# First MoE of a three-stage kernel: where the down products, the low part of the weights' sums and the copies of y stand in each engine's order

## The reference, cut to what matters

```python
attn = attention(q, k, v, tau)                # 32 heads of 576 x 64, thresholded softmax
x = attn.transpose(0, 2, 1, 3).reshape(2304, 512)
a = x @ w_a                                   # first MoE: 512 -> 1536, twice
b = x @ w_b
y = a * b @ w_out                             # 1536 -> 512
h = y @ w_in                                  # second MoE: 512 -> 1024
solu = h * softmax(h)
out = (layernorm(solu) * g_ln) @ w_out2       # 1024 -> 512
```

## Time and profile before

| | |
|---|---|
| median of 3 executions | 1001.8 us (1001.01 to 1002.4) |
| the profiled execution | 1002.01 us |
| its span, first to last instruction | 999.8 us |
| PE busy | 953.1 us (95%) |
| DVE busy | 806.3 us (81%) |
| POOL busy | 631.4 us (63%) |
| ACT busy | 509.5 us (51%) |
| first MoE, chunks 1 to 4, on PE | from 381 to 780 us |

### The profile page before, as it was taken

How to read it: one execution, slowest core, us unless ns; L and a number is a source line. 1 busy time by engine, 2 the same in 40 slices (tenths; PEclk the granted TensorE clock), 3 DMA queues, 4 the chain that set the end, 5 groups by cost and what they waited for, 6 DMA issues and landing times.

```text
span 999.8 us, 18862 instructions
## 1 busy us (share of the span) xinstructions
PE 953.1 (95%) x6222; PEld 877.2 (88%) x6222; DVE 806.3 (81%) x1298; ACT 509.5 (51%) x823; POOL 631.4 (63%) x570
## 2 busy tenths in 40 slices
PE   5999999999999998998899989998999989999998
PEld 4999999999998997998899879997999777888886
DVE  6788788878778577888788877888899778888884
ACT  3777777777778554333433343334343643333332
POOL 2777777777778346777467756775888654443320
PEclk9999999999999999999899999999999999999999
DMA  6666666666763843221311131213210200000001
GB/s 176 160 161 164 157 157 157 159 161 159 168 150 101 235 159 89 67 82 65 84 63 63 63 92 59 79 63 129 82 65 22 85 1 32 32 21 21 21 21 43
DMA packets 55676, 96.66 MB, mean 97 GB/s; under 512 B 15576, under 2 KB 24408, under 8 KB 55632
## 3 DMA queue, kind: packets, MB, share of 16 engines
q1 hardware_dynamic: 55632, 96.10, 35.1%
HBM read 58.41 MB, written 5.32 MB: 64 GB/s over the span
## 4 chain that ended last, share of the span: by engine, by line
PE 82%; DVE 8%; ACT 3%; DMA 3%; issue 2%; POOL 1%; SPq 1%; DVEq 0%; POOLq 0%; ACTq 0%
PE PS L1654 12%; PE PS L1616 8%; PE PS L1681 8%; PE PS L1618 8%; PE PS L1683 8%; PE PS L1682 8%; PE PS L1776 4%; PE PS L1777 4%; PE PS L1778 4%; PE PS L1857 3%; PE PS L1859 3%; PE PS L1858 3%; PE PS L1800 2%; PE PS L1802 2%; PE PS L1801 2%
## 5 line engine op out<-in xcount | busy, mean ns | idle before, releaser
L660 POOL TENSOR_TENSOR p_lo<-prob,p_hi 128x576 fp32r<-128x576 f32 x144 | 208.7, 1451 | 49.9 <-ACT p_hi L853 48.0
L1681 PE MATMUL PS<-x_parts,w_parts 128*128 128x256 f32 x672 | 198.1, 295 | 20.3 <-DVE w_parts L1353 20.3
L1616 PE MATMUL PS<-ops 128*128 128x288 f32 x642 | 181.6, 304 | 14.4 <-DVE ops L1269 6.7
L1683 PE MATMUL PS<-x_parts,w_parts 128*128 128x256 f32 x672 | 193.5, 288 | 0.0
L1682 PE MATMUL PS<-x_parts,w_parts 128*128 128x256 f32 x672 | 193.4, 288 | 0.0
L1618 PE MATMUL PS<-ops 128*128 128x288 f32 x642 | 177.0, 297 | 0.0
L1189 DVE TENSOR_REDUCE neg_max<-PS 128x1 f32<-128x576 f32 x144 | 108.4, 755 | 59.7 <-PE PS L1618 59.6
L1681 PEld LDWEIGHTS PS<-x_parts,w_parts 128*128 128x128 f32 x672 | 132.4, 197 | 25.0 <-issue 18.2
L1616 PEld LDWEIGHTS PS<-ops 128*128 128x128 f32 x642 | 122.2, 190 | 23.3 <-issue 12.0
L728 POOL TENSOR_TENSOR w_parts<-w_raw,w_parts 128x768 fp32r<-128x768 f32 x48 | 90.5, 1885 | 80.1 <-ACT w_parts L980 80.1
L1682 PEld LDWEIGHTS PS<-x_parts,w_parts 128*128 128x128 f32 x672 | 132.6, 197 | 1.5
(11 more groups left out here) (170 smaller groups left out, 2287.7 us busy)
## 6 DMA issues: line engine op xcount, KB each, us to landing
w_raw<-w_ab_dram SPq DMA_DIRECT2D x60, 512.0 KB, 3.4
qk_raw<-qkT_dram SPq DMA_DIRECT2D x32, 288.0 KB, 3.0
ops<-qk_hi SPq DMA_DIRECT2D x62, 144.0 KB
ops<-qk_hi SPq DMA_DIRECT2D x31, 288.0 KB
ops<-qk_lo SPq DMA_DIRECT2D x62, 144.0 KB
v_raw<-v_tiles_dram SPq DMA_DIRECT2D x32, 160.0 KB, 2.7
xT<-head_sb SPq DMA_DIRECT2D x32, 144.0 KB, 3.1
out_dram<-o_sb SPq DMA_DIRECT2D x18, 256.0 KB, 2.0
```

The source lines that it names most:

```text
L660: pool.tensor_tensor(p_lo[:, s, :], prob[:, s, :], p_hi[:, r, :].bitcast(F32), ALU.subtract).then_inc(p_lo_done, 1)
L1616: pe.matmul(ps[:, b, 0:HALF], weights[0][:, r, own], moving[0][:, r, cols], start=(n == 0), stop=False)
L1681: pe.matmul(up_ps(bank, half), w[:, 0, :], x[:, 0, :], start=(k == 0), stop=False)
L1683: ins = pe.matmul(up_ps(bank, half), w[:, 1, :], x[:, 0, :], start=False, stop=(k == 1))
```

## The change

Nothing is computed otherwise; instructions change places.

- **PE**: `down(c, 11)` goes behind `up(c + 1, 0)` of the next chunk. `down(c, 8)` is cut into two halves (two banks each), one behind `up(c, 9)`, the other behind `up(c, 10)`. `down(c, 9)` and `down(c, 10)` stay behind `up(c, 11)`. Chunk 0 keeps its order but for its `down(0, 11)`.
- **DVE**: `low_sums` of the next tile stands behind the third of the nine operations of `products`, instead of behind the ninth. At f = 11, `low_x_block(., 0)` and `low_x_sums(., 0)` stand ahead of `low_gates`.
- **ACT**: at f = 11, `high_x_block(., 1)` stands ahead of `high_gates`, with part 0.
- **ACT and DVE**: `y_out(c - 1)` follows the gate of tile 0 of chunk c.
- **PE, ACT, DVE**: chunk 1 is written out, the loop runs over chunks 2 and 3.
- **Hand-over**: ACT does three blocks of `high_wout` ahead of `expo_step(0, 0)` instead of six, two ahead of the last `y_out`, two behind the copy that follows, one behind `high_normed(0, 0)`. POOL's `low_wout` is spread in a like way.

```diff
@@ POOL
-            low_wout(range(5))
+            low_wout(range(3))
             low_y(1, (0, 1))
+            low_wout(range(3, 4))
             pool.wait_ge(half_set, 1)
             rstd(0, 0)
             low_y(1, (2, 3))
-            low_wout(range(5, 7))
+            low_wout(range(4, 7))
@@ ACT, later_step
                 if f == NF - 1 and not final:
                     high_x_block(c + 1, 0)
+                    high_x_block(c + 1, 1)
                 high_gates(c, f)
+                if f == 0:
+
+                    y_out(c - 1)
                 if f == NF - 1 and not final:
-                    for part in range(1, 4):
-                        high_x_block(c + 1, part)
+                    high_x_block(c + 1, 2)
+                    high_x_block(c + 1, 3)
                     high_blocks(c + 1, 1)
@@ ACT, loops
-            y_out(0)
-            with act.Fori(1, NCH - 1) as c:
+            for f in range(NF):
+                later_step(1, f)
+            with act.Fori(2, NCH - 1) as c:
                 for f in range(NF):
                     later_step(c, f)
-                y_out(c)
@@ ACT, hand-over
-            high_wout(range(6))
+            high_wout(range(3))
             act.wait_ge(y_done, LAST + 9)
             expo_step(0, 0)
             high_y(1, (0,))
             act.wait_ge(y_done, LAST + 10)
             expo_step(0, 1)
             high_y(1, (1, 2))
-            high_wout(range(6, NK2))
+            high_wout(range(3, 5))
             y_out(NCH - 1, range(NK))
             copy_first(1)
+            high_wout(range(5, 7))
 
             act.wait_ge(wout_lo, 2)
             high_normed(0, 0)
+            high_wout(range(7, NK2))
@@ DVE, products
                 done(dve.tensor_tensor(up_3[:, :], up_ps(1, 1), up_2[:, :], ALU.add))
+
+                if f + 1 < NF:
+                    low_sums(c, f + 1)
+                elif not (isinstance(c, int) and c == LAST_CHUNK):
+                    low_sums(c + 1, 0)
                 dve.wait_ge(up_part, 3 * m + 3)
@@ DVE, later_step
                 products(c, f)
-                if f + 1 < NF:
-                    low_sums(c, f + 1)
-                    low_gates(c, f)
-                elif not final:
+                if f == NF - 1 and not final:
                     low_x_block(c + 1, 0)
-                    low_gates(c, f)
-                    low_sums(c + 1, 0)
                     low_x_sums(c + 1, 0)
+                low_gates(c, f)
+                if f == 0:
+                    y_out(c - 1)
+                if f == NF - 1 and not final:
                     low_x_sums(c + 1, 1)
                     low_x_block(c + 1, 1)
-                else:
-                    low_gates(c, f)
@@ PE
-            def down(c, f, split=False):
+            def down(c, f, split=False, ms=range(NK)):
...
+            def chunk(c, split=False, last=False):
+
+
+                for f in range(NF):
+                    up(c, f)
+                    if f == 0:
+                        down(c - 1, NF - 1, split)
+                    elif f < NF - 3:
+                        down(c, f - 1)
+                    elif f < NF - 1:
+                        half = (f - (NF - 3)) * NK // 2
+                        down(c, NF - 4, ms=range(half, half + NK // 2))
                 if not last:
-                    for f in range(NF - 3, NF):
-                        down(c, f, split)
+                    for f in range(NF - 3, NF - 1):
+                        down(c, f)
```

More of the change, by code:

```diff
@@ L1034, in _ @@
                     high_x_block(1, 0)
+                    high_x_block(1, 1)
+                    high_sums(1, 0)
                 high_gate(f)
@@ L1038, in _ @@
                     high_wo(f + 2)
-            high_x_block(1, 1)
-            high_sums(1, 0)
             high_x_block(1, 2)
@@ L1319, in first_gate, with low_sums @@
                 dve.tensor_tensor(gate[:, 0:H], gate[:, 0:H], PS[:, 2 * (f % 2) + 1, 0:H], ALU.mult).then_inc(g_done, 1)
+            def low_sums(c, f):
+                m = NF * (c - 1) + f
+                dve.wait_ge(w_hi_done, NF + 2 * m + 2)
+                dve.tensor_tensor(w_parts[:, f % 2, 1, 3:7, :], w_raw[:, f % RAW, :, :],
+                                  w_parts[:, f % 2, 0, 3:7, :].bitcast(F32), ALU.subtract).then_inc(w_sum_lo_done, 1)
             def products(c, f):
@@ L1348, in products @@
                 done(dve.tensor_tensor(up_ps(3, 0), second, up_ps(3, 0), ALU.mult))
[L1350 to L1354, removed]
             def sum_x(c, step):
@@ L1420, in _ @@
                     low_x_block(1, 0)
+                    low_x_sums(1, 0)
+                    low_sums(1, 0)
                 low_gate(f)
@@ L1426, in _ @@
                     low_wo(f + 2)
-            low_x_sums(1, 0)
-            low_sums(1, 0)
             low_x_sums(1, 1)
             low_x_block(1, 1)
-            y_out(0)
-            with dve.Fori(1, NCH - 1) as c:
+            for f in range(NF):
+                later_step(1, f)
+            with dve.Fori(2, NCH - 1) as c:
                 for f in range(NF):
                     later_step(c, f)
-                y_out(c)
             def low_win(b):
@@ L1771, in down @@
                     at_least(pe, y_out_dve, (NK // 2) * c)
-                for m in range(NK):
+                for m in ms:
                     bank = PS[:, 4 + m, 0:width(c)]
@@ L1778, in down, with first_chunk @@
                     ins = pe.matmul(bank, w[:, 1, :], high, start=False, stop=(f == NF - 1))
-                ins.then_inc(y_done, 1)
+                if ms[-1] == NK - 1:
+                    ins.then_inc(y_done, 1)
+            def first_chunk():
+                for f in range(NF):
+                    if f > 0:
+                        first_up(f)
+                    if 1 <= f < NF - 2:
+                        down(0, f - 1, split=True)
+                for f in range(NF - 3, NF - 1):
+                    down(0, f, split=True)
             def chunk(c, split=False, last=False):
                 for f in range(NF):
[L1783 to L1788, removed]
+                    up(c, f)
[6 more added lines that the diff above has]
+                        down(c, NF - 4, ms=range(half, half + NK // 2))
                 if not last:
-                    for f in range(NF - 3, NF):
-                        down(c, f, split)
+                    for f in range(NF - 3, NF - 1):
+                        down(c, f)
             def product_of(p, a, b, bank, first=False):
@@ L1863, in _ @@
             pe.wait_ge(mask_done, SLOTS * PAIRS)
-            chunk(0, split=True)
-            with pe.Fori(1, NCH - 1) as c:
+            first_chunk()
+            chunk(1, split=True)
+            with pe.Fori(2, NCH - 1) as c:
                 chunk(c)
```

## The result

The changed kernel takes 991.4 us (median of 4 executions, 989.5 to 992.3) against 1001.4 before (of four executions now, where 1001.8 was of three): ratio 0.9896, 95% interval 0.9879 to 0.9914. The profiled execution took 991.5 us, its span is 989.4 against 999.8. A second set of six executions on another chip gave 0.9911 (0.9889 to 0.9932). The forecast was 990.5.

A forecast was written before the change was run, and what follows sets the result against it. PE's waits for low_sums, its loop with it and half clock were taken to bound the first MoE: 35.1 us to win, less 21.4 new waits, 4.3 clock, plus 2.3, less 0.4, is 11.3, giving 990.5 us; range 984.5 to 997.

The forecast's parts named there:

- Plain steps to 7.79 us, 3.5 us: In the first MoE's 35 plain steps: each falls from 7.88 to 7.79 us, winning 3.5 us.
- low_sums at 1.22 us, not 2.18: On VectorE in plain steps: at its new place low_sums meets no GpSimd operation and takes 1.22 us, not 2.18.
- the lock's: VectorE and GpSimd take a port pair exclusively per instruction, so low_sums takes 1.22 us; shared bandwidth would mean 2.18.
- third rival: At boundaries: all four half-clock cases come, 995.4 us, or low_sums takes 2.18 at eight new waits, 998.2; chance 0.19.
- a sign of being wrong: In plain steps: the prediction called itself wrong if GpSimd's adds still collide; no size given.
- A wait of 1.4 at f = 11: Before the third pair of f = 11: PE waits 1.4 us for the gate, four times, 5.6 us.
- 0.3 and 2.35 at f = 1: At three chunk boundaries: PE waits 0.3 us at f = 1's second pair, 2.35 at its third; 8.0 us.
- Chunk 1's start, 7.0: From chunk 0 to 1: waits of 1.2 and 0.8 before up(1,0), 2.65 and 2.35 in up(1,1); 7.0 us.
- New waits 21.4: In the first MoE: new PE waits of 7.0, 8.0, 5.6 and 0.8 total 21.4 us.
- Clock, 4.3 us lost: Behind the new waits: TensorE at half clock after two or three of four, 1.7 us each, 4.3 us lost.
- The end, 2.3 less 0.4: At the hand-over: PE's wait for the y copies falls by 2.3 us; less covered last products cost 0.4.
- second rival: In 36 steps: the weight chain sets the pace at 14.7 us over PE's 13.4; 1037 us; chance 0.04.

The follow-up runs named there:

- e1: Changed kernel with low_sums put back behind the ninth operation of products for every f; 985.8 us, 0.9856 of the kernel before.
- e3: Changed kernel with low_sums behind the ninth operation of products at f = 0 alone; 981.9 us, 0.9814 of the kernel before.
- Edit 3: y_out(c - 1) put behind the gate of tile 0, chunk 1 written out; forecast to cost nothing; not timed as a whole.
- e6: Kernel before with only chunk 1 written out on PE, ACT and DVE; 1002.3 us, 1.0002 of the kernel before.
- edit 4: The hand-over's new order of high_wout and low_wout, part of the changed kernel (991.4 us); undone there, 994.9 us.
- e2: Changed kernel with the old hand-over order of high_wout and low_wout; 994.9 us, 0.9942 of the kernel before.
- e8: As e4, with copy_product(4, 11) ahead of the high parts of T1 and two parts of y; 978.5 us, 0.9769 of before.
- e4: Changed kernel with low_sums behind the ninth operation of products at f = 0 and 1; 979.4 us, 0.9785 of the kernel before.
- edit 1: low_sums moved behind the third operation of products; alone on the kernel before, 995.8 us, 0.9946 of it.
- e9: As e4, with the old hand-over order of high_wout and low_wout; 983.0 us, 0.9820 of the kernel before.
- e10: e4 run once more, unchanged, beside later kernels; 979.1 us, 0.9772 of the kernel before.

## Why the prediction was right, step by step

- **Plain steps to 7.79 us, 3.5 us.** Right: 7.78 and 7.79.
- **low_sums at 1.22 us, not 2.18.** Right, median 1.225. The choice between the two ends was the lock's, and e1 shows both in one edit: moved back, 2.18 again. At the boundaries, where the third rival feared for it, GpSimd's L728 gave way instead: 2.15 us long at 488.42, beside low_sums' 1.23 at 487.64; the longest of the 48 low_sums is 1.34. GpSimd's adds do still collide in some steps, a sign of being wrong by the prediction's words, but with sums of x; those steps keep their 7.78 us. By the Trainium skill ("SBUF — State Buffer", "SBUF: two separate sides") the port pair is held for a whole instruction by VectorE with two SBUF inputs or by GpSimd; the trace agrees: before, L728 ended at 454.01 and low_sums, begun at 452.91, at 455.09, 1.08 behind it.
- **A wait of 1.4 at f = 11.** Measured by starts 1.30, 1.23, 1.23 and 1.30 beyond the 0.12 of a matmul: 5.1 for 5.6.
- **0.3 and 2.35 at f = 1.** Measured 0.25 and 2.14, 2.14 and 2.28. VectorE's idle of 4.13 us is the one forecast as 4. That low_sums' place at f = 0 is the cause is shown by e3.
- **Chunk 1's start, 7.0.** Measured 1.1, 0.7, 2.5 and 1.2: 5.5. The last is 1.2 short: the twelve matmuls of the pair before it ran at half clock and took 1.2 us longer, which came off the wait.
- **New waits 21.4** were thus about 18.5 with the 0.6 in step 10 of the last chunk.
- **Clock, 4.3 us lost.** Too little: the mean of 0.993 over 989.4 us is 6.9 us of work lost, against 10.0 before by the same sum. Behind the waits of 2.1 to 2.5 the clock was at half at all four boundaries of the profiled execution, 3.4 us each, not at two or three. This is the mis-sized term, 2.6 us too small; the waits, 2.9 too large, nearly cancel it, and that is luck. The trace of before had a third wait of 2.7 us, at 575.30, that the prediction did not count; the clock was at half behind it as well, so it was two of three:

```profile
572.00:580.00 8.00, 5.46 (x35) 5.26 (x34) 5.79 (x10) 2.13 (x4) 5.21 (x4) 0.79 0.19 66
```

  The four executions' clocks were 0.991 to 0.996, their spans 990.2 to 987.4.
- **Edit 3 free.** Right for the chunk written out (e6). The copies of y behind f = 0 were not tried alone; in the trace PE waits for none of them in the first MoE.
- **The end, 2.3 less 0.4.** 1.8 us in the trace (216.1 to 214.4 behind the last up()), but of 3.0 won by edit 4 and 1.2 lost otherwise (e2's 217.3 against 216.1): both terms were too small, and here too the errors cancel. That the 1.2 are the late last products is shown in part, by the 0.6 that e8 wins back.

The second rival (steps set by the weight chain) did not come; of the third, the clock half came, at 1.7 us for each stretch and not at the 2.3 that it had put.

## What to carry to other kernels

Moving an operation earlier on an in-order engine puts everything behind it into series with that operation's inputs. It may pay in the steady steps and cost at the loop's ends, where the input is late; there the old place can be kept for just those iterations (e4). A gain that was worked out as waits removed should be checked for what waits in their place, and each edit should be tried alone as well as undone. Here edit 1 won 5 us alone and cost 4 among the others.

## What the runs showed of the hardware that was not expected

- Behind waits of 2.1 to 2.5 us PE was at half clock for 3.4 us, where before the change it was not behind one of 2.7. In e9 it was behind one of 2.1 at the turn, in e2 not behind one of 2.6 at the same place. It differs for one wait of one kernel too: at chunk 1's start PE waits 2.33 us in e4 and 2.32 in e10, and these are the windows round it, e4, then e10:

```profile
390.00:398.00 8.00, 6.11 (x34) 5.95 (x35) 5.12 (x11) 4.33 (x8) 5.15 (x6) 0.79 0.25 75
```
```profile
390.00:398.00 8.00, 7.10 (x48) 6.61 (x49) 7.19 (x15) 3.98 (x8) 6.25 (x6) 1.00 0.19 66
```

- The same program differs between executions in this: mean clocks of 0.988 to 0.996 in ten executions of the changed kernel. With the waits for the gate at f = 1 gone, they were 0.997 to 0.999 (e10).
